# The experts' first product, formed by columns in two halves of 64 rows instead of by rows and then turned

## The reference

```python
# 1. attention: 4 batches x 8 heads, 576 positions, head width 64, block-causal mask (blocks of 64)
scores = scale * q @ k.T ; mask ; softmax ; attn @ v
# 2. feed-forward: x (2304 x 512), w_in (512 x 2048), w_out (2048 x 512)
h = x @ w_in;  g = where(h > 0, h, exp(min(h, 0)) - 1);  x = g @ w_out
# 3. experts: w_gate (512 x 8), w1 (8 x 512 x 1024), w2 (8 x 1024 x 512)
do_compute = x @ w_skip > 0
e_idx = argmax(xc @ w_gate);  gate_w = softmax(xc @ w_gate)[e_idx]      # xc: the rows that compute
for e in range(8):
    h = maximum(xc[mask_e] @ w1[e], 0)
    y[mask_e] = gate_w * (h @ w2[e])
out = x;  out[do_compute] = xc + y
```

## Time and profile before

| | |
|---|---|
| median of 3 runs | 790.11 us |
| the profiled execution | 791.72 us, its span 789.9 us |
| TensorE busy, share of the span | 758.0 us, 96% |
| VectorE, ScalarE, GpSimd busy | 66%, 44%, 31% |
| mean granted TensorE clock | 0.993 of full speed |
| experts, from the turn of x for tile 1 to the end of the span | 597.57 to 789.9 us |

### The profile page before, as it was taken

One profiled execution on the slowest core, in us unless ns is written; L12 is line 12 of the kernel. 1 busy time (PEld: TensorE's weight loads), 2 busy tenths in 40 slices (PEclk: granted clock), 3 DMA queues, 4 the chain that ended last, 5 costly groups with the idle time before them and its releaser, 6 DMA issues.

```text
span 789.9 us, 15565 instructions
## 1 busy us (share of the span) xinstructions
PE 758.0 (96%) x5170; PEld 639.8 (81%) x5171; DVE 524.1 (66%) x1331; ACT 347.8 (44%) x830; POOL 245.3 (31%) x240
## 2 busy tenths in 40 slices
PE   5999999899999999999999999999987999999995
PEld 3777777688998888898988998888865777887884
DVE  3888888954337974984797598436665997367342
ACT  3888888644322213223222322324452774446231
POOL 4888887944501201210121021000112231222211
PEclk9999999999999999999999999999998999999998
DMA  9556677462422112101210200502424898174000
GB/s 163 133 149 157 163 162 188 144 198 61 147 79 103 48 57 91 50 21 62 59 41 0 90 22 27 214 0 81 135 95 126 270 340 303 46 229 153 34 15 9
DMA packets 101061, 88.15 MB, mean 112 GB/s; under 512 B 63812, under 2 KB 78532, under 8 KB 100880
## 3 DMA queue, kind: packets, MB, share of 16 engines
q1 hardware_dynamic: 95584, 81.89, 34.7%
q0 software_dynamic: 3056, 5.00, 1.9%
q10 hardware_dynamic: 2368, 0.59, 0.4%
HBM read 72.26 MB, written 18.34 MB: 115 GB/s over the span
## 4 chain that ended last, share of the span: by engine, by line
PE 86%; ACT 5%; DVE 4%; issue 3%; DVEq 1%; DMA 1%; POOL 0%; SPq 0%; ACTq 0%; POOLq 0%
PE h_ps L1733 12%; PE out_ps L1733 12%; PE h_ps L1734 12%; PE h_ps L1735 12%; PE out_ps L1735 11%; PE out_ps L1734 11%; PE o_ps L684 5%; PE s_ps L668 3%; ACT prob L541 3%; PE t_ps L593 2%; PE out_ps L1869 1%; PE s_ps L663 1%; ACT pt L525 1%; PE tr_ps L1834 1%; DMA raw_qk<-in_q_dram 1%
## 5 line engine op out<-in xcount | busy, mean ns | idle before, releaser
L1558 ACT ACTIVATE ex<-h_ps 128x384 f32<-128x384 f32 x96 | 47.3, 493 | 272.3 <-PE h_ps L1735 272.3
L1733 PE MATMUL h_ps<-xt_hi,wi_hi 128*128 128x384 f32 x384 | 131.8, 343 | 0.0
L1734 PE MATMUL h_ps<-xt_lo,wi_hi 128*128 128x384 f32 x384 | 129.7, 338 | 0.0
L1735 PE MATMUL h_ps<-xt_hi,wi_lo 128*128 128x384 f32 x384 | 129.7, 338 | 0.0
L1394 DVE TENSOR_SCALAR ex<-ex 128x384 f32<-128x384 f32 x96 | 36.9, 385 | 131.1 <-ACT ex L1558 129.7
L1733 PE MATMUL out_ps<-wo_hi,gt 128*128 128x512 f32 x288 | 114.5, 398 | 0.0
L1735 PE MATMUL out_ps<-wo_hi,gt 128*128 128x512 f32 x288 | 113.9, 396 | 0.0
L1734 PE MATMUL out_ps<-wo_lo,gt 128*128 128x512 f32 x288 | 113.3, 393 | 0.0
L541 ACT ACTIVATE prob<-s_ps,negmax 128x128 f32<-128x128 f32 (+2 forms) x144 | 77.8, 556 | 14.1 <-DVE negmax L399 13.7
L1276 DVE CUSTOM_DVE_ANT_0 x2t<-x,w_raw 128x512 bf16<-128x512 f32 x108 | 82.7, 806 | 0.4
L1172 POOL TENSOR_TENSOR xt_lo<-x_raw,xt_hi 128x384 fp32r<-128x384 f32 x20 | 28.3, 1413 | 157.8 <-ACT xt_hi L1575 157.5
(11 more groups left out here) (180 smaller groups left out, 1589.0 us busy)
## 6 DMA issues: line engine op xcount, KB each, us to landing
w_raw<-in_moe_w_dram SPq DMA_DIRECT2D x56, 512.0 KB, 5.2
raw_qk<-in_q_dram SPq DMA_DIRECT2D x32, 144.0 KB, 3.2
attn_t<-attn_sb SPq DMA_DIRECT2D x16, 288.0 KB, 2.2
x_raw<-attn_t SPq DMA_DIRECT2D x24, 192.0 KB, 2.4
w_raw<-recip_rows SPq DMA_DIRECT2D x48, 96.0 KB, 2.8
out_dram<-x SPq DMA_DIRECT2D x18, 256.0 KB, 2.1
x_rows<-x SPq DMA_DIRECT2D x18, 256.0 KB, 2.6
v<-in_v_dram SPq DMA_DIRECT2D x32, 128.0 KB, 2.9
```

The source lines that it names most:

```text
L1558: act.activation(ex[:, f % 2], h_ps[:, f % 2, 0:NB], ACT.Exp).then_inc(ex_done, 1)
L1733: pe.matmul(dst, stat[0], mov[0], start=start, stop=False, skip_group_check=True)
L1734: pe.matmul(dst, stat[0], mov[1], start=False, stop=False, skip_group_check=True)
L1735: return pe.matmul(dst, stat[1], mov[0], start=False, stop=stop, skip_group_check=True)
```

## The change

The first product of a tile is now formed by columns: the stationary operand is a piece of w1, the moving one is x, so the result has 128 hidden columns as partitions and 128 tokens along the row. It comes out in the shape that the second product needs, and `turn_h` is gone. Each product is cut in two halves of the contraction: rows 0 to 63 of a chunk k go to bank `h_ps[:, j]`, rows 64 to 127 to bank `out_ps[:, j]` (`hm_ps[j][s]`), as separate matmuls one behind the other. A tile has 2 halves j x 4 chunks k x 4 column blocks f x 3 terms x 2 row halves s = 192 such matmuls, each with a stationary operand of 64 x 128 and 128 moving columns.

The two banks are added behind it: ScalarE copies the second bank to `h_sb` (`h_copy`), VectorE adds the first (`h_sum`), ScalarE writes the ReLU of the sum as the high part (`ht_high`), and VectorE makes the low part as max(h, 0) - high in one instruction (`ht_low`). The order on TensorE becomes hidden(t, 0), hidden(t, 1), turn_x(t+1), output(t), with nothing of the tile before in between. `next_w1` in an expert's first tile moves behind all of the tile's own steps on both engines, and the waits for w2's low parts move into `output`, two chunks at a time.

```diff
-        xt_ps, hm_ps, ht_ps, y_ps = tr_ps, h_ps, out_ps[:, 0:HALVES], out_ps[:, HALVES]
+        xt_ps, y_ps = tr_ps, out_ps[:, HALVES]
+        hm_ps = [[ps[:, j, :] for ps in (h_ps, out_ps)] for j in range(HALVES)]
...
+            def h_sum(t, j):
+                dve.wait_ge(hc_done, HALVES * t + j + 1)
+                dve.tensor_tensor(h[:, j], hm_ps[j][0], h[:, j], ALU.add).then_inc(hs_done, 1)
             def ht_low(t, j):
                 dve.wait_ge(ht_hi_done, HALVES * t + j + 1)
-                dve.tensor_tensor(ht[1][...], ht_ps[:, j]..., ht[0][...].bitcast(F32), ALU.subtract)
+                dve.scalar_tensor_tensor(ht[1][...], h[:, j]..., 0.0, ht[0][...].bitcast(F32),
+                                         ALU.max, ALU.subtract).then_inc(ht_lo_done, 1)
...    # VectorE, first(): behind the split of w2
                     row(t)
-                    next_w1(dve, e, i, w1_low, [0])
+                    h_sum(t, 0)
                     ht_low(t, 0)
-                    next_w1(dve, e, i, w1_low, [1])
+                    h_sum(t, 1)
                     xt_low(t + 1)
-                    next_w1(dve, e, i, w1_low, [2, 3])
+                    ht_low(t, 1)
+                    next_w1(dve, e, i, w1_low, range(PIECES))
...    # ScalarE
-            def relu(t, j):
-                wait(act, ht_done, HALVES * t)
+            def h_copy(t, j):
                 act.wait_ge(hm_done, HALVES * t + j + 1)
-                act.activation(h[:, j * BANK:(j + 1) * BANK], hm_ps[:, j], ACT.Relu)
+                if not is_zero(t):
+                    act.wait_ge(ht_lo_done, HALVES * (t - 1) + j + 1)
+                act.activation(h[:, j], hm_ps[j][1], ACT.Copy).then_inc(hc_done, 1)
             def ht_high(t, j):
-                act.wait_ge(ht_done, HALVES * t + j + 1)
-                if not is_zero(t):
-                    act.wait_ge(ym_done, t)
-                act.activation(ht[0][...], ht_ps[:, j]..., ACT.Copy)
+                act.wait_ge(hs_done, HALVES * t + j + 1)
+                act.activation(ht[0][...], h[:, j]..., ACT.Relu).then_inc(ht_hi_done, 1)
             def other(e, i, t):     # first(): the same, behind the split of w2, next_w1 at its end
+                h_copy(t, 0); ht_high(t, 0); h_copy(t, 1); xt_high(t + 1); ht_high(t, 1)
...    # TensorE
             def hidden(e, i, t, j, ks=range(KC)):
...
-                    last = mm3(hm_ps[:, j], [x[:, k, :] for x in mxt],
-                               [w[:, k, j * BANK:(j + 1) * BANK] for w in w1_sb[i]],
-                               k == 0, k == KC - 1)
+                    for f in range(KC):
+                        for c, (a, b) in enumerate(((0, 0), (0, 1), (1, 0))):
+                            for s in range(2):
+                                rows = slice(s * P // 2, (s + 1) * P // 2)
+                                last = pe.matmul(hm_ps[j][s][:, f * P:(f + 1) * P],
+                                                 w1_sb[i][a][rows, k, (j * KC + f) * P:(j * KC + f + 1) * P],
+                                                 mxt[b][rows, k, :], start=k == 0 and f == 0 and c == 0,
+                                                 stop=k == KC - 1 and c == 2, skip_group_check=True)
...
-            def turn_h(t, j):
...
-            def tile(e, i, t, before, ask=lambda: None):
-                if before is not None:
-                    outputs(before, t - 1)
+            def tile(e, i, t):
                 hidden(e, i, t, 0)
-                if before is not None:
-                    output(before, t - 1, range(EARLY, FCE))
-                ask()
-                hidden(None, i, t, 1, range(TURN_K))
-                turn_h(t, 0)
-                hidden(None, i, t, 1, range(TURN_K, KC))
+                hidden(None, i, t, 1)
                 turn_x(t + 1)
+                output(e, i, t)
```

More of the change, by code:

```diff
@@ L1485, in first @@
                     for j in range(HALVES):
+                        h_sum(0, j)
+                    for j in range(HALVES):
                         ht_low(0, j)
@@ L1500, in first @@
                     row(t)
-                    next_w1(dve, e, i, w1_low, [0])
+                    h_sum(t, 0)
                     ht_low(t, 0)
-                    next_w1(dve, e, i, w1_low, [1])
+                    h_sum(t, 1)
                     xt_low(t + 1)
-                    next_w1(dve, e, i, w1_low, [2, 3])
+                    ht_low(t, 1)
+                    next_w1(dve, e, i, w1_low, range(PIECES))
                 ask()
             def other(e, i, t):
-                if not is_zero(e):
-                    ht_low(t - 1, 1)
                 row(t)
+                h_sum(t, 0)
                 ht_low(t, 0)
+                h_sum(t, 1)
                 xt_low(t + 1)
-                if is_zero(e):
-                    ht_low(t, 1)
+                ht_low(t, 1)
             finish_attention = attend["vector"](dve)
@@ L1721, in _ @@
             soften(LAST, 1)
-            relu(0, 0)
+            h_copy(0, 0)
             soften(LAST, 2)
-            relu(0, 1)
+            h_copy(0, 1)
             over_experts(act, first, other)
-            total = all_tiles(act)
-            ht_high(total - 1, 1)
         @block.tensor
@@ L1850, in hidden, with output @@
                 if ks[-1] == KC - 1:
                     last.then_inc(hm_done, 1)
[L1853 to L1857, removed]
+            def output(e, i, t):
+                pe.wait_ge(final_done, t + 1)
+                for f in range(FCE):
                     if f % KC == 0:
                         pe.wait_ge(ht_lo_done, HALVES * t + f // KC + 1)
+                    if e is not None and f % (FCE // PIECES) == 0:
+                        pe.wait_ge(w2_lo, PIECES * e + f // (FCE // PIECES) + 1)
@@ L1860, in output @@
                     last = mm3(y_ps, [x[:, f, :] for x in ht], [w[:, f, :] for w in w2_sb[i]],
                                f == 0, f == FCE - 1)
-                if FCE - 1 in chunks:
-                    last.then_inc(ym_done, 1)
-            def turn_h(t, j):
[L1866 to L1877, removed]
-            def tile(e, i, t, before, ask=lambda: None):
-                if before is not None:
-                    outputs(before, t - 1)
-                hidden(e, i, t, 0)
-                if before is not None:
-                    output(before, t - 1, range(EARLY, FCE))
-                ask()
-                hidden(None, i, t, 1, range(TURN_K))
-                turn_h(t, 0)
-                hidden(None, i, t, 1, range(TURN_K, KC))
+                last.then_inc(ym_done, 1)
@@ L1890, in tile @@
+            def tile(e, i, t):
+                hidden(e, i, t, 0)
+                hidden(None, i, t, 1)
                 turn_x(t + 1)
+                output(e, i, t)
             def first(e, i, t, ask):
                 if is_zero(e):
-                    turn_h(0, 0)
-                    turn_h(0, 1)
-                    output(0, 0, range(FCE))
+                    output(0, 0, 0)
                     turn_x(1)
                     pe.wait_ge(route, ROUTED)
-                    ask()
                 else:
-                    pe.wait_ge(w2_lo, PIECES * e)
@@ L1902, in first @@
-                    tile(e, i, t, None if is_one(e) else 1 - i, ask)
+                    tile(e, i, t)
+                ask()
             def other(e, i, t):
-                if is_zero(e):
-                    tile(None, i, t, None)
-                    outputs(i, t)
-                    output(i, t, range(EARLY, FCE))
-                else:
-                    pe.wait_ge(w2_lo, PIECES * (e + 1))
-                    tile(None, i, t, i)
+                tile(None, i, t)
             def first_hidden(f):
@@ L1940, in _ @@
             over_experts(pe, first, other)
-            pe.wait_ge(w2_lo, PIECES * E)
-            total = all_tiles(pe)
-            outputs((E - 1) % 2, total - 1)
-            output((E - 1) % 2, total - 1, range(EARLY, FCE))
 _INS = ['q', 'k', 'v', 'moe_w_in', 'moe_w_out', 'moe2_w_skip', 'moe2_w_gate', 'moe2_w1', 'moe2_w2']
```

43 lines of the change are left out of this document (14 added, 29 removed).

## The result

The changed kernel takes **908.28 us** (median of 4 runs, 907.35 to 908.69) against 790.89 for the kernel before on the same chip (4 runs, 790.05 to 792.07): a ratio of 1.148 [1.1465, 1.1495]. It is slower, as forecast, but by 117 us and not by 70: the range ended at 890. The profiled execution took 908.29 us, its span is 906.5.

The account below looks back on a forecast made before the run. TensorE was taken to bound the kernel, busy 96% of the span. Thirteen periods +57.8, tile 1 +5.1, tile 0 +7.5 and the end -0.4 made +70 us, forecast 861 us, range 848 to 890.

Parts of the forecast that it names:

- The pair: Two half-height first-layer matmuls side by side on TensorE: 0.112 us, set by the weight load; 96 a tile, 10.8 us.
- The period: One expert tile, from one turn of x to the next: 17.2 us against 12.73; thirteen of them +57.8 us.
- the steps between shapes: TensorE going from 128-row to 64-row matmuls and back: 0.2 us a step, 0.4 a tile, ends 0 and 0.7.
- No row of line 1869: Sign in the profile after: the turns of h, 0.87 us a tile on TensorE, are gone.
- no wait for the low part of h: Output on TensorE: half 1's ScalarE and VectorE chain stays hidden by some 0.4 us; otherwise at most 0.5 a tile.
- A sum of two banks: VectorE's added work in each half of a tile: 0.69 us, 1.4 a tile, hidden under the products.
- the moved splits: w1 halves behind the tile's own work on VectorE, 4.9 us: find room under 10.8 us of products, cost 0.
- tile 1: Second expert tile: +5.1 us, with the low clock there taken to halve either form alike and left out.
- tile 0: First expert tile, within the routing: products, shape steps and VectorE's sums delay the count and lists, +7.5 us, ends 5 and 9.
- instruction supply: Rival, with ScalarE's and VectorE's chain and shape steps: 1 to 2 us a tile more, 876 to 891 us; 9%.
- The clock drops because the array is half idle: Rival on the expert pairs, with halves not running side by side: 0.22 us or more a pair, about 1017 us; 5%.
- the other side's rival: Half-height loads are cheap: 0.063 us a pair, period 12.5, total 791 us, no change or a little faster; 4%.

Follow-up runs that it names:

- full height with fillers: Changed kernel with one 128-row matmul per pair, plus 512-column filler products in waits of tiles 0 and 1: 857.0 us, 1.0861 to the kernel before.
- experiment 3: Changed kernel with 256 moving columns instead of 128 in every half-height matmul: 886.15 us, 1.121 to the kernel before.
- experiment 2: Changed kernel at full height: one 128-row matmul in place of each pair, 96 a tile, no fillers: 866.59 us, 1.0963 to the kernel before.

## Why the prediction was off

**Right.** The pair: 0.112 us taken, 0.112 measured. The period: 17.18 against 17.05; 0.4 for the steps between shapes against 0.32. "No row of line 1869", no wait for the low part of h from tile 1 on, and turns 17 us apart in clean periods are all there. A sum of two banks costs 0.69 us on VectorE (L1467, x30) and hides, as do the moved splits, but for waits of 0.2 and 0.6 us in the periods of 17.61 and 17.72. The sum comes near where nothing stalls: at full height with fillers the median is 857.0 us and the profiled execution 851.8; 15 tiles of 0.32 more give 861.8 and 856.6 for the same with half height, against 861.7 by the sum. That it meets the median so closely is luck, since with the fillers tile 1 takes 12.9 us where the sum has 15.8, and tile 0 isn't as forecast either. (Of the arithmetic, 791.72 + 70 less 1.6 is 860, and the forecast says 861; nothing hangs on it.)

**The step that failed** is in the sum, at tile 1: "The clock is down there for a few us (granted 0.68); it halves either form alike, and I leave it." The sum put the clock's cost at nothing there, in tile 0 and in the thirteen periods. The second term that failed is instruction supply, held as a rival of at most 2 us a tile. Of the span's growth of 116.6 us, 70 were forecast. The other 46.6 (tile 0 counted from its own turn of x, 570.86 us now and 571.63 before):

| | forecast | measured | more |
|---|---|---|---|
| tile 0 | +7.5 | 39.17 - 25.94 = +13.2 | 5.7 |
| tile 1 | +5.1 | 22.94 - 10.65 = +12.3 | 7.2 |
| the two stalls' periods and the one behind each | 4 x 17.18 | 33.89 + 19.37 + 29.61 + 18.84 = 101.7 | 33.0 |
| the other nine periods | 9 x 17.18 | 156.9 | 2.3 |
| start and end | -0.4 | -2.0 | -1.6 |

The stalls themselves are 4.35 + 2.15 + 2.09 + 1.18 = 9.8 us of the 33; the other 23 are the clock behind them. Tile 0's 5.7 are the clock as well, by an estimate: its pairs run for 12.20 us at 0.50 (583.30 to 595.50), at a pace of 0.21 in place of 0.11, some 6 us more than at the full clock, and the count, VectorE's lists and tile 1 wait behind them. At full height tile 0 took 38.8 us where the clock fell among its products, and 33.7, with fillers, where it held.

So the low clock does not halve either form alike. In the kernel before, 5 us of 512-wide products passed in tile 1 before the clock was back, so it pays once: 0.68 over 10.65 us is some 6.8 us at half speed. In the narrow form some 19 us of pairs passed at 0.50, and the clock was back only in the output behind them. The mechanism was in reach: the clock of 0.68 in tile 1 was read, but it wasn't asked how long it would stay down in the new form.

**The rivals.** "The clock drops because the array is half idle" came closest, and was argued away with attention's full clock. Those scores are 256 wide, and experiment 3 shows in the experts' products that the width makes the difference, and experiment 2 that the height doesn't. It is not as the rival had it, with 0.22 or more for every pair: the periods from 740.81 to 791.97 hold 1.00 with the narrow pairs. There no gap comes ahead of them. But a gap isn't needed: in tile 0 the clock fell at 583.15 with no gap since 571, in the pairs among the routing's short products (lengths 0.27, then 0.41, pace 0.11, then 0.21). It fell there at 579.4 to 584.4 in three of the four other traces with 128 columns and three terms, and held in the fourth, full height with fillers. The fall in the changed kernel:

```profile
583.04 0.29 PE L1848 MATMUL h_ps<-m_xt_lo,wi_hi 64*128 64x128 f32 x1
583.15 0.39 PE L1848 MATMUL h_ps<-m_xt_hi,wi_lo 64*128 64x128 f32 x1
583.35 0.41 PE L1848 MATMUL h_ps<-m_xt_hi,wi_hi 64*128 64x128 f32 x1
```

Of the other side's rival nothing came: a half-height load costs what a full one does. The Trainium skill ("TensorE: Matmul & The Clock Gate", LDWEIGHTS) was the rule that spoke against the change, and the trace agrees to 5%: 0.112 us a pair against the prediction's estimate of 107 ns from that page.

**Open.** Why the clock doesn't come back under the narrow stream wasn't separated; only that with the same stream, twice as wide, it did. Why it falls in tile 0 in most executions and not in all is open too. Each long branch has a fetch of instructions inside it, but why it lasts 4.87 us in one turn and 3.70 in the next, while the packets took 1 to 2.4 us, and what decides which forward branch is long, isn't shown. Of tile 1's 7.2 us most is the clock (18.9 us of pairs at half speed are some 9 us more, where the kernel before lost some 3); the rest wasn't taken apart.

## What to carry to other kernels

Price a matmul of this type by its load when fewer than some 256 columns stream behind it, and ask of each weight load how many columns it serves. Ask of each gap on TensorE which products follow it: here 2 us of waiting cost 12 to 14 us in all where narrow products followed, and 2.7 us of waiting were followed by 6.8 us at half speed, some 3 us lost, where 512-wide ones did. When a loop body grows fourfold in instructions, look at the branches in the sequencer's records and at the instruction fetches before trusting any sum of durations. And when an edit that should only fill a gap changes the program's length, look whether the stalls have moved.

## What the runs showed of the hardware

- No branch on TensorE in the experts' part takes over 0.25 us with 60 matmuls a tile in the loop, or over 0.46 with 92 or 124. With 220 most take under 0.5, but two to four in each trace take 3.3 to 5.0 us, each with an instruction fetch inside it; such packets are 29 in the kernel before and 54 to 57 here.
- A long branch costs nothing where enough matmuls were issued ahead of it: 3.36 us from 672.96 in the changed kernel, with no gap over 0.9 us behind it.
- A `float32r` matmul with 128 moving columns is held to no slower rate than a wide one: pairs take 0.112 and full-height ones 0.11, the load's pace. At 256 columns the pair takes 0.118, so there loading and streaming cost about the same.
- Two 64-row matmuls side by side load in the time of one, 0.11 us, and a single 128-row load takes the same.
- The 1.2 GHz level can last 24 us while TensorE is 100% busy by the profile (702.70 to 726.51: busy 23.81 of 23.81 us, clock 0.50).
